# A three-block transformer kernel: the first batch of attention placed operation by operation, its values as three products on 64 columns, a minimum moved to GpSimd

## What is computed

```
scores = causal(q @ k.T / sqrt(D));  a = softmax(scores)          # per batch and head
local  = a @ v
q_p    = phi(q)                                                    # phi(x) = (x if x > 0 else exp(x) - 1) + 1
mem    = (q_p @ M_prev) / (q_p @ z_prev + 1e-6)
x      = g * mem + (1 - g) * local;  g = sigmoid(beta)             # heads side by side: 2304 x 512
x      = silu(x @ w_in) @ w_out                                    # 512 -> 2048 -> 512
h      = x @ w2_in;  s = h * softmax(h)                            # 512 -> 1024
out    = layernorm(s) * g_ln @ w2_out                              # 1024 -> 512
```

## Time and profile before

| what | us |
|---|---|
| median of 3 runs | 875.06 |
| lowest and highest | 874.63, 880.20 |
| the profiled execution | 880.67 |
| its span, from first to last instruction | 878.8 |
| around the span | 1.9 |
| attention alone, until the first unit of chunk 0 | 0 to 114.0 |
| chunk 0, chunk 1, chunk 2 with attention woven in | 114.0 to 259.4, to 395.9, to 526.7 |
| rest | 526.7 to 878.8 |

### The profile page before, as it was taken

How to read it: one execution, slowest core, us unless ns; L and a number is a source line. 1 busy time by engine, 2 the same in 40 slices (tenths; PEclk the granted TensorE clock), 3 DMA queues, 4 the chain that set the end, 5 groups by cost and what they waited for, 6 DMA issues and landing times.

```text
span 878.8 us, 13106 instructions
## 1 busy us (share of the span) xinstructions
PE 830.0 (94%) x4576; PEld 704.0 (80%) x4576; DVE 523.1 (60%) x1003; ACT 405.0 (46%) x897; POOL 328.0 (37%) x350
## 2 busy tenths in 40 slices
PE   3977799999899999999999999999999999999998
PEld 2655678877788888878888879999998888888886
DVE  4777665677675575675475543154426666666764
ACT  3676666666656555555655434334121222222222
POOL 3667647586545444544544324133120000000000
PEclk8788779999999999999999999999999999999999
DMA  6222237666675455455444337433300000000001
GB/s 174 60 81 63 57 122 237 217 217 194 226 253 171 141 186 169 142 167 170 153 151 158 122 130 307 138 121 120 130 15 4 22 24 24 24 24 24 24 13 37
DMA packets 67480, 105.63 MB, mean 120 GB/s; under 512 B 29024, under 2 KB 40288, under 8 KB 67168
## 3 DMA queue, kind: packets, MB, share of 16 engines
q1 hardware_dynamic: 67120, 104.85, 37.3%
q10 hardware_dynamic: 304, 0.05, 0.0%
HBM read 83.38 MB, written 21.50 MB: 119 GB/s over the span
## 4 chain that ended last, share of the span: by engine, by line
PE 78%; DVE 6%; DMA 4%; ACT 4%; POOL 3%; SPq 2%; issue 2%; ACTq 0%
PE banks L1355 20%; PE banks L1343 19%; PE banks L1413 11%; PE banks L1482 11%; PE banks L1292 5%; PE banks L1320 4%; PE banks L1249 2%; DMA wr_raw<-in_w_out 2%; PE banks L1471 2%; DVE pt_lo L984 1%; DVE neg_max L970 1%; PE banks L1254 1%; SPq L493 1%; DMA z_row<-in_z_prev 1%; ACT prob L715 1%
## 5 line engine op out<-in xcount | busy, mean ns | idle before, releaser
L1355 PE MATMUL banks<-g_hi,wr 128*128 128x512 f32 (+1 forms) x640 | 198.7, 378 | 3.3 <-POOL g_lo L641 2.1
L624 POOL TENSOR_SCALAR prob<-prob,inv_sum,gate_all 128x576 f32<-128x576 f32 (+2 forms) x144 | 96.3, 680 | 111.3 <-DVE inv_sum L978 111.3
L1355 PEld LDWEIGHTS banks<-g_hi,wr 128*128 128x128 f32 x640 | 119.2, 189 | 19.5 <-issue 4.8
L1343 PE MATMUL banks<-xc_hi,wr 128*128 128x512 f32 x384 | 130.2, 405 | 0.8 <-DVE x_t L1029 0.8
L1355 PE MATMUL banks<-g_lo,wr 128*128 128x512 f32 (+1 forms) x320 | 118.1, 369 | 0.0
L984 DVE TENSOR_TENSOR pt_lo<-banks,pt_hi 128x512 fp32r<-128x512 f32 x144 | 83.3, 586 | 45.6 <-ACT pt_hi L721 44.8
L715 ACT ACTIVATE prob<-banks,neg_max 128x576 f32<-128x576 f32 (+2 forms) x144 | 78.3, 548 | 33.3 <-DVE neg_max L970 28.9
L641 POOL TENSOR_TENSOR g_lo<-gu,g_hi 128x512 fp32r<-128x512 f32 x48 | 61.9, 1290 | 82.9 <-ACT g_hi L761 82.9
L721 ACT ACTIVATE pt_hi<-banks 128x512 fp32r<-128x512 f32 x144 | 74.6, 520 | 36.3 <-PE banks L1292 33.7
L697 POOL TENSOR_TENSOR st<-st 128x1 f32<-128x1 f32 x18 | 9.9, 551 | 210.2 <-DVE st L1166 210.2
L1343 PEld LDWEIGHTS banks<-xc_hi,wr 128*128 128x128 f32 x384 | 73.5, 191 | 16.0 <-DVE x_t L1029 1.3
(11 more groups left out here) (126 smaller groups left out, 1784.7 us busy)
## 6 DMA issues: line engine op xcount, KB each, us to landing
wr<-split_w SPq DMA_DIRECT2D x96, 512.0 KB, 3.4
split_w<-wr SPq DMA_DIRECT2D x32, 512.0 KB, 4.6
k_raw<-in_k_t SPq DMA_DIRECT2D x16, 288.0 KB, 3.1
out<-o SPq DMA_DIRECT2D x18, 256.0 KB, 2.0
q_raw<-in_q_t SPq DMA_DIRECT2D x16, 256.0 KB, 2.7
vm_raw<-in_v_main SPq DMA_DIRECT2D x16, 256.0 KB, 2.6
wr_raw<-in_w_in SPq DMA_DIRECT2D x16, 256.0 KB, 3.8
wr_raw<-in_w_out SPq DMA_DIRECT2D x16, 256.0 KB, 4.0
```

What stands on the lines that cost most here:

```text
L624: pool.tensor_scalar(pr, pr, inv_sum[p % 2][:, columns(t, h)], gate, ALU.mult, ALU.mult).then_inc(prob_done, 1)
L1343: mm = pe.matmul(out_bank, w[:, a, k], x[:, k], start=(i == 0), stop=(i == 3 * KC - 1))
L1355: mm = pe.matmul(out_bank, w[:, a, k], g, start=(i == 0), stop=(i == 11))
```

## The change

- **Attention alone** now has 1040 small steps, and each operation of each pair stands at a step of its own, in tables written out for pairs 0 to 5 (`SCORES_AT`, `MAX_AT`, `EXPS_AT`, ...). The same operations run on the same engines; their order on each engine, and how far pairs overlap, follow from the tables. Before the first unit of chunk 0 TensorE now also has unit `phi03`, values part 0 of pair 4 and two score tiles of pair 5.
- **Second buffers for pairs 0 to 3** (`BATCH = 4`) of `q_raw`, `k_raw`, `vm_raw`, `vm` and `prob`, placed in memory that the feed-forward block uses later; two more clears on VectorE at the start. Three more loads are issued at the start, the first six weight loads only at step 145.
- **Values of pairs 0 to 3**: three products on 64 columns (v_hi with the high and the low part, v_lo with the high part), summed in PSUM. The result needs one copy: ScalarE copies head 1, VectorE head 0, where each of the four parts had a copy on ScalarE and an add on VectorE.
- **phi**: GpSimd takes min(q, 0) for all 16 pairs; ScalarE keeps the Exp.
- **Woven steps**: chunk 0 has 35 steps instead of 36, with idle steps (18, 28, 30), chunk 1 (11, 20, 29, 31), chunk 2 (2, 18, 30, 31). The tail scores come one step earlier (-1 for 0), turn `8b` at 5 for 6, `phi` at 9 for 10, value parts at 10, 13, 14, 14 for 10, 11, 14, 15, `v_high` at 6 for 8, `v_low` and `load_v` at 10 for 9, `q_low` at 3 for 4. On ScalarE the exponentials stand behind `g_high`; on GpSimd `q_low` and `g_low` come first, the normalisations last.

```diff
-STEPS = 9
-SCORES = {0: 4, 1: 3, 3: 2, 5: 1}
+FIRST = 1040
+LASTSTEP = FIRST + STEPS * (NP - BATCH) + 2 * STEPS
+WOVEN_FROM = FIRST - 11
+MAX_AT = steps([[99, 107, 137, 171], [211, 239, 280, 342], [423, 436, 465, 531], [563, 616, 640, 666], [729, 798, 862,
+                     918], [987, 1040, 1042, 1044]], [0, 2, 4, 6])
+EXPS_AT = steps([[108, 133, 143, 158, 178, 193, 200, 207, 213], [251, 267, 282, 295, 303, 358, 369, 376, 383], [432,
...
+                     [1, 2, 2, 4, 4, 7, 7, 7, 8])
+NORMS_AT = steps([[124, 163, 171, 198, 205, 232, 237, 243, 248], [283, 330, 338, 346, 353, 398, 404, 410, 415], [459,
+PARTS_AT = steps([[282, 311, 356, 381], [472, 501, 554, 589], [669, 698, 743, 779], [858, 887, 932, 967], [1037, 1042,
+                     1043, 1043], [1048, 1051, 1052, 1052]], [10, 13, 14, 14])
+CHUNK_STARTS = [WOVEN_FROM + STEPS * BATCH * c + after for c, after in enumerate((11, 10, 10, 10))]
+IDLE = ((18, 28, 30), (11, 20, 29, 31), (2, 18, 30, 31))
...
+            def phi_low(i):
+                pool.wait_ge(qn_in, 80 * (i + 1))
+                if i > 1:
+                    pool.wait_ge(turned, len(UNITS) * (i - 2) + UNITS.index("phi03") + 1)
+                pool.tensor_scalar(phi[i % 2][:], qn_raw[:], 0.0, None, ALU.min).then_inc(phi_min, 1)
...
+                if p < BATCH:
+                    at = x_cols(p)
+                    act.activation(x_t[D:P, at + lo:at + hi], bank[VALUE_BANKS[h]][0:D, 0:hi - lo], ACT.Copy).then_inc(x_done, 1)
+                    return
...
+                if p < BATCH:
+                    dve.wait_ge(pv_done, len(PARTS) * p + n + 1)
+                    dve.tensor_copy(x_t[0:D, at + lo:at + hi], bank[VALUE_BANKS[h]][0:D, 0:hi - lo]).then_inc(x_done, 1)
+                    return
...
+            def value_terms(p):
+                if p < BATCH:
+                    return D, ((slice(0, 1), pt_hi), (slice(0, 1), pt_lo), (slice(1, 2), pt_hi))
+                return P, ((slice(0, 2), pt_hi), (slice(0, 2), pt_lo))
```

More of the change, by code:

```diff
@@ L125, in exps_of @@
[L125 to L143, removed]
@@ L462, in w_loads, with stores @@
             return 16 * (unit // NW + 1)
+        def stores(unit):
+            return 16 * sum(x % NW == unit % NW and is_split(x) for x in range(unit + 1))
         def y_place(m, at, n):
@@ L650, in _ @@
                 w = woven(s - 1)
+                for i, e in NORMS_AT.get(s, ()):
+                    normalise(i, e)
+                for i, _ in PHI_MIN_AT.get(s, ()):
+                    phi_low(i)
+                for i, _ in PHI_Z_AT.get(s, ()):
+                    phi_times_z(i)
+                for i, _ in PHI_LAST_AT.get(s, ()):
+                    phi_last(i)
+                for i, part in V_LOW_AT.get(s, ()):
+                    v_low(i, part)
+                if first_pass(s, W_LOW_EARLY) is not None and MLP[first_pass(s, W_LOW_EARLY) % NM][0] == "H":
+                    w_low(first_pass(s, W_LOW_EARLY))
@@ L684, in _ @@
-                if pair_at(s, 4, 1):
-                    q_low(pair_at(s, 4, 1))
+                for i, _ in PHI_MIN_AT.get(s, ()):
+                    phi_low(i)
+                for i, _ in PHI_Z_AT.get(s, ()):
+                    phi_times_z(i)
+                for i, _ in PHI_LAST_AT.get(s, ()):
+                    phi_last(i)
+                for i, part in V_LOW_AT.get(s, ()):
+                    v_low(i, part)
+                if first_pass(s, W_LOW_EARLY) is not None and MLP[first_pass(s, W_LOW_EARLY) % NM][0] == "H":
+                    w_low(first_pass(s, W_LOW_EARLY))
@@ L798, in _ @@
             for s in range(FIRST):
-                turns, w = units_of(s), woven(s - 1)
-                if w and MLP[w[1]][0] == "H":
-                    g_high(h_index(w[0], MLP[w[1]][1]))
-                for q, e in exps_of(s):
-                    exp_tile(q, e)
+                turns, w = HIGHS_AT.get(s, ()), woven(s - 1)
+                for i, e in EXPS_AT.get(s, ()):
+                    exp_tile(i, e)
+                if turns:
+                    unit_hi(*turns[0])
+                for i, u in turns[1:]:
+                    unit_hi(i, u)
+                for i, n in HALVES_AT.get(s, ()):
+                    half_up(i, n)
                 if w and MLP[w[1]][0] == "H":
```

773 lines of the change are left out of this document (408 added, 365 removed), and 14 rows, old and new, of tables (EXPS_AT, HIGHS_AT, LOWS_AT, NORMS_AT).

## The result

| kernel | median, us | ratio to before, 95% interval |
|---|---|---|
| changed | 887.0 (885.7 to 888.2) | 1.0117 (1.0077 to 1.0157) |
| changed, ScalarE's two phi passes back | 861.6 (860.7 to 863.6) | 0.9844 (0.9807 to 0.9881) |

The change costs 1.2%, where 868.9 us and a range from 860 to 880 were forecast. One part of it, the minimum on GpSimd, costs 25 us. The rest wins 13.5, more than twice the 6.2 of the forecast, and the second row of the table is the fastest kernel here.

What follows compares the result with a forecast made beforehand. The prediction took TensorE to bound the kernel (94% busy), with attention alone bound by hand-overs. Its terms 2.4 + 3.8 + 1.5 - 1.5 = 6.2 us took 875.06 to 868.9 us, range 860 to 880.

Steps and rivals of the forecast that it cites:

- part 1: Attention alone, before chunk 0: tables read as times, 18.9 us a pair for 20.6, GpSimd's minimum hidden; gain 2.4 us.
- part 4: Woven steps: the last exponential behind `g_high` on ScalarE delays the next pair's tail scores on TensorE; loss 1.5 us.
- Part 2: Before chunk 0: TensorE work moved there shortens its list in the three woven chunks; gain 3.8 us.
- Part 3: Chunk 0: `v_high` two steps earlier and `q_low` in front cut its 8.9 us excess; gain 1.5 us.
- The slower one: First batch: TensorE at half clock becomes the bound, third product costs 3.2 us a pair; 884.1 us, chance 0.12.
- the better first batch: Attention alone: TensorE runs ahead of the tables, spacing 17.2 instead of 18.9 us a pair; 862.1 us, chance 0.18.

Runs made afterwards that it cites:

- one-step run: Changed kernel with GpSimd's minimum one step earlier from pair 6 on (-5 for -4), ScalarE's Exp where it was: 875.8 us, ratio 0.9996.

## Why the prediction was wrong

The step that failed is in part 1: the minimum "costs nothing; without that cover 4 x 0.92 = 3.7 us", and its repeat for the woven part, "costed at nothing". Four things were wrong in it.

- **The price.** 0.92 us was scaled from `normalise`, "the same instruction at nearly this size". It is the same opcode with another pair of operations. Alone it takes 1.81 us. The bounds given, 0.74 to 2.1, held that and not the 2.3 of the woven part; the value chosen was near the wrong end. No row of before showed this form of the instruction.
- **The cover.** It was read from GpSimd's free time (36 of 98.5 us). Free time covers an instruction that may come early. This one has a window and no slack: in the first stage its input lands late, in the woven part its consumer stands in the same step, and ScalarE's in-order list stands at the Exp, with `tanh` behind it. The rule that a wait added to a list is asked after (what is queued behind it, who waits for that) was applied to the exponentials of part 4 and not to this wait. The one-step run (11.2 us) shows it for the new order of the woven steps; in the kernel before, with its own order, the same step cost chunks 1 and 2 nothing.
- **The load.** ScalarE's pass used to meet the load of the queries at the Exp's place, with 6.1 us of waits, nearly all at the start. The tables put the minimum 16 to 71 steps ahead of the Exp, on the engine whose `q_low` and product with z release SP's next loads. The prediction has no term for that wait or for the loop that it closes.
- **The start.** Nothing ahead of the first maximum "is changed in kind". It came at 17.13 and not at 15.48, and at 15.63 with ScalarE's passes: the first minimum, 1.83 us against 0.74, is ahead of phi's add and so of the maximum on VectorE. That is 1.5 us before anything else.

Without the minimum the steps can be judged one by one. From the timelines of after and of the kernel with ScalarE's passes, maximum first and the memory product of pair 3 second:

```profile
17.13 0.76 DVE L1058 TENSOR_REDUCE neg_max<-banks 128x1 f32<-128x576 f32 x1
...
103.49 0.53 PE L1419 MATMUL banks<-pt_hi,vm 64*64 64x320 f32 x2
```

```profile
15.63 0.76 DVE L1055 TENSOR_REDUCE neg_max<-banks 128x1 f32<-128x576 f32 x1
...
91.25 0.53 PE L1416 MATMUL banks<-pt_hi,vm 64*64 64x320 f32 x2
```

- **Part 1, tables as times: the numbers came out without the minimum, the cause is not shown.** Forecast: maximum near 15.6, pair 3 near 91.4, spacing 18.9. With ScalarE's passes: 15.63, 91.25 and, from pair 0's 34.99, (91.25 - 34.99) / 3 = 18.75. With the minimum the spacing is (103.49 - 36.07) / 3 = 22.5, longer than the 20.6 of before. The first unit of chunk 0 came at 107.8 for the 111.5 worked out: part 0 of pair 4 began at 105.99, where 5.6 + 103.7 = 109.3 was said, so the end of the batch ran ahead of its table. That this is the work of the tables isn't shown: the value form alone, without any table, gave 19.2 us a pair and the first unit at 109.9. The prediction had the spacing from the tables and nothing of it from the value form, so its agreement may be luck.
- **Part 2, work out of the way: borne out.** With ScalarE's passes chunk 0 is TensorE's alone at 132.6 us, and the 136.5 us of chunk 1 before less that is 3.9, for 3.8 forecast (3.6 with the 136.2 of the table of first units).
- **Part 3, chunk 0's excess: mis-sized.** All 8.9 us went, for 1.5 forecast, also the part of the clock that was left out: the chain has the first 12 matmuls of the first unit at full clock, for the 7.93 us of 24 in the earlier trace rows.

```profile
107.99 2.85 PE banks L1451 x12
```

  `v_high` was named as the cause, and its places have no effect that could be told. The order within the steps gives 3.9 to 6.8 us and the value form some of it. SP's wait for `v_low` fell from 54.7 to 5.4 us in after and in the kernel with ScalarE's passes alike, so that it fell is no proof that it paid.
- **Part 4, exponentials behind `g_high`: no such loss.** Taken as a loss of 1.5 us. TensorE's waits for an exponential in the woven part are 0.2 us in all in after, and with ScalarE's passes it is busy throughout chunks 0 and 1, so nothing is lost there. The order of which this place is a part wins 3.9 to 6.8 us. That it does so by what now stands earlier (`g_high` feeds `g_low` and a unit of TensorE's) is an argument and was not tested.
- **The value form** was given no more than 0.9 us of VectorE's and as much of ScalarE's time a pair, within the tables. It wins 4.1 us with the tables and 5.4 without.
- **The rivals.** The slower one was TensorE at half clock with the third product on the path, 884.1 us. The measured 887.0 is near it, but not by its mechanism: the granted clock of the first stage is 0.94 and 0.83 in after where it was 0.67 and 0.69, and the form with the third product wins. The sum of 862.1 for the better first batch is near the 861.6 measured without the minimum, but by chunk 0 and not by the spacing it was for.

The Trainium skill, "SBUF — State Buffer", section "Who interferes with whom", was weighed in the forecast as holding VectorE up for each minimum. The trace doesn't show that. `k_lo` takes 949 ns on the mean ahead of chunk 0 in after and 1170 with ScalarE's passes. In chunks 0 to 2, in the same order:

```profile
L1033 DVE SCALAR_TENSOR_TENSOR k_lo<-k_raw,k_hi 128x576 fp32r<-128x576 f32 x10 | 16.8, 1678 | 0.0
```

```profile
L1030 DVE SCALAR_TENSOR_TENSOR k_lo<-k_raw,k_hi 128x576 fp32r<-128x576 f32 x10 | 16.9, 1688 | 0.0
```

The minimum does not lengthen it; the long woven `k_lo` is there without it, beside `g_low`. It is the minimum that gets longer: 1.81 us alone and in the first stage, 2.30 or 2.31 all ten times in the woven part, where it starts while a `k_lo` begun before it still runs (133.58 to 135.32 us at the first place). One step earlier, where no `k_lo` runs beside it, the same ten take 1.80 to 2.02 us.

**What stays open:** where the 5 us of before's profiled executions lie; which engine's order within the steps wins; and how much the tables of the first batch give by themselves, for which no run was made (what the value form, 4.1 to 5.4, and the order, 3.9 to 6.8, leave of the 13.5 us is 1.3 to 5.5, if they add up); why ScalarE's waits for the minimum cost the chunks in the new order and not in the old; and how the 12.5 us of the first stage part into the wait for the load, the instruction's length and the late start.

## What to carry to other kernels

An engine's idle time covers an added instruction only if its input is there early and its consumer late: look up when the input lands, and what stands behind the consumer in its own list, before you call it free. Look up too who releases that input: if it is the engine that will wait for it, the wait feeds itself. Put producer and consumer on different engines at least one step apart; here that one number was worth 11 us, and the ten instructions themselves about 2 or less. A wait in a trace is not yet a price: 43.8 us of the same waits cost the kernel before nothing in its later chunks. Take the price of a GpSimd instruction from a row with the same operations, not the same opcode.

## What the hardware showed

- GpSimd's `tensor_scalar` on 128 x 640 float32: 0.72 to 0.88 us for two multiplies, 1.81 for a single operation (also a single multiply) by a constant, 1.88 by a pointer (a scalar read from memory), 2.35 for minimum and multiply by constants, 2.50 for pairs by pointers with a minimum or an add. More arithmetic can be the shorter instruction. A multiplying `tensor_tensor` of this size takes 1.25, so less than a minimum against a constant.
- VectorE did the same minimum in 0.47 to 0.49 us at best, 1.13 on the mean of all 16 (1.55 at most places in the woven part). The Trainium skill, "GPSIMD Engine Reference", section "4.1 Engine selection", calls GpSimd with one input "roughly line-rate"; the trace disagrees for this operation, 1.81 against 0.49 us.
- At 128, 512 and 640 elements the single minimum takes 0.52, 1.49 and 1.81 us alone, some 2.5 ns an element and 0.2 us around it. In the woven part the minimum of 128 takes 1.03 us and that of 640 2.31, both 0.5 more than alone.
